# Attention: the turn of the keys put ahead of the first weighted sums, its second part one step on, high queries and back-turning a step up

## The reference, cut to what matters

```python
q_pool = q.reshape(B, H, S // 2, 2, D).mean(axis=3)        # B=4, H=8, S=1152, D=64
scores = scale * np.matmul(q_pool, k.transpose(0, 1, 3, 2))
scores = scores - np.max(scores, axis=-1, keepdims=True)
attn = np.exp(scores)
attn = attn / (np.sum(attn, axis=-1, keepdims=True) + 1e-09)
return np.matmul(attn, v)                                   # 32 heads, 576 x 1152 scores each
...
x = attn_out as rows of 512 numbers                         # 2304 rows
x = moe(x)                                                  # 8 experts, with a skip gate
return moe2(x)                                              # 8 experts, with an output gate
```

## Time and profile before

| what | value |
|---|---|
| median of 3 runs | 1257.56 us |
| profiled execution, its own time | 1266.61 us |
| its span, first to last instruction | 1264.8 us |
| mean granted TensorE clock | 0.952 of full speed |
| head after head, where nothing disturbs | 19.1 us |
| busy in the span: PE, DVE, ACT, POOL | 89%, 60%, 43%, 34% |

### The profile page before, as it was taken

How to read it: one execution, slowest core, us unless ns; L and a number is a source line. 1 busy time by engine, 2 the same in 40 slices (tenths; PEclk the granted TensorE clock), 3 DMA queues, 4 the chain that set the end, 5 groups by cost and what they waited for, 6 DMA issues and landing times.

```text
span 1264.8 us, 21764 instructions
## 1 busy us (share of the span) xinstructions
PE 1128.5 (89%) x7630; PEld 923.3 (73%) x7630; DVE 762.5 (60%) x1710; ACT 545.0 (43%) x945; POOL 435.6 (34%) x335
## 2 busy tenths in 40 slices
PE   6899998889898889988994699999949999999996
PEld 4666676666665666756673699999938999999996
DVE  6565666566667566675655377667654555656551
ACT  2455554445554455443543344444414334443420
POOL 0566555476565666546665100000000000000000
PEclk9799998899999999998998799999978999999998
DMA  4162222132222322223115671318485427141100
GB/s 117 47 190 66 66 58 66 38 97 65 66 50 64 86 66 65 58 57 85 29 30 200 231 276 41 134 59 291 169 319 185 139 85 277 50 159 50 33 17 13
DMA packets 74396, 132.57 MB, mean 105 GB/s; under 512 B 11040, under 2 KB 29472, under 8 KB 74320
## 3 DMA queue, kind: packets, MB, share of 16 engines
q10 hardware_dynamic: 26240, 69.22, 15.2%
q1 hardware_dynamic: 43424, 50.58, 14.8%
q0 software_dynamic: 4656, 11.79, 2.7%
HBM read 106.12 MB, written 19.24 MB: 99 GB/s over the span
## 4 chain that ended last, share of the span: by engine, by line
PE 79%; DVE 13%; ACT 3%; issue 3%; DMA 1%; SPq 1%; POOL 0%; POOLq 0%; another core or an unknown queue 0%; DVEq 0%; ACTq 0%
PE PS L706 22%; PE PS L570 9%; PE PS L491 9%; DVE mx L997 6%; PE PS L553 6%; PE PS L540 6%; PE PS L719 6%; PE PS L720 6%; PE PS L723 6%; PE PS L554 5%; DVE KA L980 2%; DVE KA L977 2%; ACT arena_p L816 1%; PE PS L583 1%; PE PS L607 1%
## 5 line engine op out<-in xcount | busy, mean ns | idle before, releaser
L442 POOL TENSOR_TENSOR arena_a<-arena_a,arena_p 128x576 f32<-128x576 f32 x224 | 323.3, 1443 | 163.6 <-ACT arena_p L816 149.7
L997 DVE TENSOR_REDUCE mx<-PS 128x1 f32<-128x384 f32 (+1 forms) x480 | 250.8, 550 | 146.6 <-PE PS L540 142.4
L706 PE MATMUL PS<-moe,W 128*128 128x128 f32 x2432 | 282.9, 278 | 1.5 <-ACT moe L897 1.5
L706 PEld LDWEIGHTS PS<-moe,W 128*128 128x128 f32 x2432 | 280.0, 194 | 4.0 <-ACT moe L897 2.3
L816 ACT ACTIVATE arena_p<-PS 128x576 f32<-128x576 f32 x288 | 187.3, 651 | 220.1 <-PE PS L554 211.3
L553 PE MATMUL PS<-QHT,KA 128*128 128x288 f32 x576 | 194.2, 340 | 0.4 <-ACT QLT L827 0.4
L540 PE MATMUL PS<-KA,QHT 128*128 128x384 f32 (+1 forms) x480 | 179.0, 376 | 11.2 <-DVE mx L997 10.6
L570 PE MATMUL PS<-arena_p,arena_a 128*64 128x288 f32 x1152 | 170.8, 435 | 7.2 <-DVE R L1065 6.1
L554 PE MATMUL PS<-QLT,KB 65*128 65x288 f32 x576 | 174.3, 306 | 0.0
L1173 DVE TENSOR_TENSOR W2L<-W2R,W2H 128x1024 fp32r<-128x1024 f32 x148 | 171.0, 1217 | 0.7 <-ACT W2H L788 0.7
L788 ACT CAST W2H<-W2R 128x1024 fp32r<-128x1024 f32 x148 | 144.0, 1047 | 46.0 <-PE PS L723 41.3
(11 more groups left out here) (171 smaller groups left out, 1145.7 us busy)
## 6 DMA issues: line engine op xcount, KB each, us to landing
W<-in_moe_w ACTq DMA_DIRECT2D x16, 2048.0 KB, 14.3
W2R<-in_moe_w ACTq DMA_DIRECT2D x16, 2048.0 KB
moe<-xs SPq DMA_DIRECT2D x40, 258.0 KB, 4.3
arena_a<-in_k SPq DMA_DIRECT2D x32, 288.0 KB, 2.9
arena_a<-in_v SPq DMA_DIRECT2D x32, 288.0 KB, 2.8
KB<-KA SPq DMA_DIRECT2D x32, 288.0 KB, 3.1
arena_a<-in_q SPq DMA_DIRECT2D x32, 256.0 KB, 3.1
xs<-padrow ACTq DMA_DIRECT2D x8, 258.0 KB, 3.7
```

Of the source, the lines that this page charges most:

```text
L442: nc.gpsimd.tensor_tensor(Acc[u], Acc[u], P[u][:, t, :], ALU.add).then_inc(acc_step, 1)
L706: last = nc.tensor.matmul(PS[:, HB + f // 4, (f % 4) * PN:(f % 4 + 1) * PN], W1[s][:, d, f * PN:(f + 1) * PN], xT[:, d, :], start=(d == 0) ...
L997: vec.reduce_max(mx3[0:n, t, c:c + 1], PS[0:n, MXB + b % 2, 0:KB_], AX.X).then_inc(pr_max, 1)
```

## The change

Seven things move; no instruction is added or taken away, and the numbers that each computes are the same.

- TensorE: `trans_k(h+2, 0)` stands ahead of the first weighted sums in step 0; `trans_k(h+2, 1)` at the end of step 1 (it was behind the second weighted sums in step 2).
- TensorE: `trans_qh(h+2, 0)` at the start of step 3, `trans_qh(h+2, 1)` at its end (both were at step 4).
- TensorE: the third rough block of one step moves from the end of step 5 to step 4, ahead of the third weighted sums.
- TensorE: `back_values` in step 5 (was 6), `back_sums` between the two halves of step 6 (was 7), `back_logits` at the end of step 6 (was 8).
- ScalarE: `k_high` 0 and 1 and `q_high` ahead of the exponential of step 1; `k_high` 2 ahead of that of step 2; `qh_out` 0 ahead of, and `qh_out` 1 behind, that of step 3.
- VectorE: `k_low` 0 and 1 in slot 1 behind `pool_q` (were in 3 and 4), `k_low` 2 in slot 5 (was 7), `q_low` in slot 7 (was 9).

```diff
--- before.py
+++ after.py
@@ -635,47 +635,45 @@
                 now, after, before = has(h), has(h + 1), has(h - 1)
                 blocks = iter(range(NBLK))
                 for t in range(KT):
-                    if t == 4 and has(h + 2):
+                    if t == 3 and has(h + 2):
                         trans_qh(h + 2, 0)
                     if now:
                         scores(h, t, 0)
                     if after and t < 7:
                         prior(h + 1, next(blocks))
+                    if t == 6 and before:
+                        back_sums(h - 1)
                     if now:
                         scores(h, t, 1)
                     if after and t < 7:
                         prior(h + 1, next(blocks))
                     if t == 0:
+                        if has(h + 2):
+                            trans_k(h + 2, 0)
                         if before:
                             if h - 1 in RANKS_IN:
                                 pe.wait_ge(norm, HEAD_NORM * (h - 2) + 3)
                                 ranks_of_batch(RANKS_IN.index(h - 1))
                             weighted(h - 1, 0)
-                        if has(h + 2):
-                            trans_k(h + 2, 0)
-                    if t == 2:
-                        if before:
-                            weighted(h - 1, 1)
-                        if has(h + 2):
-                            trans_k(h + 2, 1)
+                    if t == 1 and has(h + 2):
+                        trans_k(h + 2, 1)
+                    if t == 2 and before:
+                        weighted(h - 1, 1)
+                    if t == 3 and has(h + 2):
+                        trans_qh(h + 2, 1)
                     if t == 4:
-                        if has(h + 2):
-                            trans_qh(h + 2, 1)
+                        if after:
+                            prior(h + 1, next(blocks))
                         if before:
                             weighted(h - 1, 2)
                             sums(h - 1)
-                    if t == 5 and after:
-                        prior(h + 1, next(blocks))
+                    if t == 5 and before:
+                        back_values(h - 1)
                     if t == 6 and before:
-                        back_values(h - 1)
-                    if t == 7:
-                        if before:
-                            back_sums(h - 1)
-                        if after:
-                            trans_ql(h + 1, 0)
-                            trans_ql(h + 1, 1)
-                    if t == 8 and before:
                         back_logits(h - 1)
+                    if t == 7 and after:
+                        trans_ql(h + 1, 0)
+                        trans_ql(h + 1, 1)
 
             pe.wait_ge(ident_set, 1)
             assert NBLK == 15 and KT == 9
@@ -846,23 +844,21 @@
             def body(h):
                 for t in range(KT):
                     if has(h + 2):
+                        if t == 1:
+                            k_high(h + 2, 0)
+                            k_high(h + 2, 1)
+                            q_high(h + 2)
+                        if t == 2:
+                            k_high(h + 2, 2)
                         if t == 3:
-                            k_high(h + 2, 2)
-                        if t == 4:
                             qh_out(h + 2, 0)
                     if has(h - 1) and t == 5:
                         o_out(h - 1)
                         s_out(h - 1)
                     if has(h):
                         exps(h, t)
-                    if has(h + 2):
-                        if t == 1:
-                            k_high(h + 2, 0)
-                            k_high(h + 2, 1)
-                        if t == 2:
-                            q_high(h + 2)
-                        if t == 4:
-                            qh_out(h + 2, 1)
+                    if has(h + 2) and t == 3:
+                        qh_out(h + 2, 1)
                     if t == 7 and has(h + 1):
                         ql_out(h + 1, 0)
                         ql_out(h + 1, 1)
@@ -1103,13 +1099,11 @@
                     if has(h + 2):
                         if b == 1:
                             pool_q(h + 2)
-                        if b == 3:
                             k_low(h + 2, 0)
-                        if b == 4:
                             k_low(h + 2, 1)
+                        if b == 5:
+                            k_low(h + 2, 2)
                         if b == 7:
-                            k_low(h + 2, 2)
-                        if b == 9:
                             q_low(h + 2)
                     if first is not None and 2 <= b < 2 + RT_STEPS[0]:
                         route_step(first, b - 2)
```

## The result

The changed kernel took 1240.22 us (median of 4 runs, 1235.36 to 1241.71) where the kernel before took 1257.79 (1255.83 to 1262.3). The ratio is 0.9849, with a 95% interval of 0.981 to 0.9888. It is faster, by some 18 to 26 us. The forecast was 1216 with a range of 1196 to 1242: the direction is right, the range holds the time close to its edge, and the gain is less than half of the 42 us forecast by the first comparison, and about 0.6 of it by the pair of traces (1264.8 to 1239.9).

What follows compares the result with a forecast made beforehand. The prediction took TensorE (89% busy) to bound the kernel, its idle time lying in the turning. It summed -1.13 us a head times 30 to -34, plus -8 in routing heads: -42 from 1257.6, about 1216, range 1196 to 1242.

Steps and rivals of the forecast that it cites:

- What bounds it, and which waits go: TensorE bounds; its waits at the ninth tile's turn (0.35 us) and high queries' turn (1.08) go, -1.43 a head.
- My sum: Per-head total of the waits: -1.13 us a head, times 30 gives -34 us.
- The 0.15 for maxima: In step 2, some 0.15 us a head of TensorE's waits for row maxima goes too.
- The copy of the low queries, +0.2: After step 7, its exponential goes ahead of the copy, so the next head's first scores start about 0.2 us late.
- The third rough block, 0: Its 0.21 us wait moves to step 4 with the block; costed at 0, bounds 0.1 gained and 0.4 lost.
- GpSimd beside the query sum, +0.25: At a head's start `pool_q` runs beside GpSimd's last addition, delaying the second key subtraction: +0.25 us a head, bounds 0 and 1.2.
- the second rival: `pool_q` pays the full 1.2 us beside GpSimd in every head: 28 us less gain, 1244 us; chance 0.14.
- The routing heads, -8 beyond the usual saving: In three stretches of three heads, some clock falls stay away: 8 of 39 us saved, bounds 0 and 35.
- Back-turning costed by itself: Moving it a step or more earlier costs 0 in waits for its copies (bounds 0 and 0.1); the low queries' copy pays +0.2.
- The slower rival: TensorE stands 1 to 1.5 us at the end of step 1, its clock falls in each head: about 1300 us; chance 0.06.
- That the clock would stay up in the routing heads: Rival: some 30 of the 39 us there go instead of 8, giving about 1193 us; chance 0.15.

Runs made afterwards that it cites:

- e2: Changed kernel with VectorE's query sum (`pool_q`) made one body earlier, for head h + 3 in slot 9: 1210.70 us, ratio 0.9662 to the kernel before.
- e4: e2 with the waits for the low queries' copy split by part: 1215.13 us, ratio 0.9617 to the kernel before; repeated as e4_again, 1217.49 us, 0.9639.
- e1: Changed kernel with GpSimd's last two additions of each head cut to 8 of 576 columns: 1207.34 us, ratio 0.9628 to the kernel before.
- e7: e4 with all GpSimd additions in the heads around the routing cut to 8 of 576 columns: 1199.97 us, ratio 0.9516 to the kernel before.
- e3: Changed kernel with the back-turning alone put back where the kernel before has it: 1256.44 us, ratio 1.0032 to the kernel before.
- b1: Kernel before with the back-turning alone moved up as in the change: 1252.54 us, ratio 0.9919 to the kernel before.

## Why the prediction was right or wrong

- **What bounds it, and which waits go: right.** The wait at the high queries' turn left every quiet head, TensorE's own work stayed, and with the query sum out of the way the head is 17.75. My sum without the GpSimd term was 19.10 - 1.43 + 0.2 - 0.15 = 17.72. The 0.15 for maxima was not tried alone, and the waits behind maxima as a whole did not shrink: 10.2 us before, 19.5 now, 15.2 in e2. So the close sum doesn't show that this term is right.
- **The copy of the low queries, +0.2: right**, 0.21 by e4.
- **The third rough block, 0: right in size.** TensorE waits 0.21 at it as before, now in step 4. It was not tried alone.
- **GpSimd beside the query sum, +0.25: the step that failed**, in size. It costs 0.66 a head (e1 and e2). I saw the mechanism and had 1.2 as its bound, but I let `pool_q` end at 2.7 to 3.0 after the head's start and the second subtraction at 4.1 to 4.4; they ended at 3.07 and 4.51. I then priced only the ninth tile's turn, which is 0.44 late against e2 and not 0.25. What I left out is the rough block behind it: its maxima stand on VectorE behind the delayed subtractions, so TensorE pays a second time, another 0.22. 0.41 x 30 = 12 us. This was the second rival in kind (VectorE beside GpSimd), at less than its full price, and its 0.14 was too little: the trace had a row of 1.67 for such an instruction, and GpSimd's backlog at the head's end was plain. The measured median lies in that rival's band (1234 to 1254), and the range holds it only because it was drawn into that band.
- **The routing heads, -8 beyond the usual saving: too much.** The excess over nine quiet heads went from 38.95 (210.85 less 9 x 19.10) to 35.7 (201.49 less 9 x 18.42), a gain of 3. The additions are again behind much of it: with the query sum out of their way (e2) the excess is 23.9 (183.62 less 9 x 17.75), 15 under before, and e7 takes 20 us out of the stretches, on e4. VectorE's routing steps now stand among tighter slots, and one was held for 1.46 us. But e4_again has an excess of 38.8 with the query sum out of the way, so these heads depend on more than that, and what it is stays open.
- **Back-turning costed by itself: wrong in kind.** I treated it as a part whose gain is nothing and whose price is 0.2. e3 shows that without it the rest loses 0.25 a head against before instead of gaining 0.68: it is what makes the keys' move pay, in a kernel whose query sum is held up (with the query sum ahead it was not tried), and b1 shows that it shortens the routing stretches alone by 13 us. The two halves can't be added.
- **The slower rival did not come:** its condition, a wait of 1 to 1.5 us at the ninth tile, was not met. With 0.28 us there the clock stayed at 1.00 through seven quiet heads. (Its own sum gives 1306, not 1300.) That the clock would stay up in the routing heads did not come either: it is 0.95, 0.93 and 0.93 after 0.86, 0.95 and 0.88.
- **The sum against the traces.** From the first to the last `divide` it went from 610.91 us (68.80 to 679.71) to 589.56 (63.09 to 652.65), by -21.4: 19 quiet spaces x -0.68 = -12.9, nine in the stretches -9.4, and the last three +0.9. The same by my sum would have been 28 x -1.13 - 8 = -39.6. Of the 18 us that are missing, 8.6 are in the quiet heads, 8.8 in the stretches and 0.9 in the last three. The rest of the span gave 3.5: 5.7 before the first `divide`, where the kernel before itself differs by 3 us between its two traces (68.80 and 65.64), less 2.2 lost behind the last.

## What to carry to other kernels

When work moves earlier on one engine, ask of each instruction what it will now run beside (here the query sum beside GpSimd's additions, 1379 ns instead of 480), and follow a delay on an in-order queue to everybody behind it, not only to the one who waits first. Move what is light and has slack (here a sum of queries, a whole body ahead) out of the contended place rather than the heavy work. And test the halves of a change apart: here each alone lengthened the quiet head, and both together shortened it.

## What was not expected of the hardware

The prediction knew that a VectorE instruction with two operands in SBUF is slow beside a GpSimd addition; how regular and how long it is was not expected. The query sum took 1379 ns in the median of 32 instances where 480 is its own length, and a routing step 1455 against 254. Two instances can be followed: L990 in the earlier trace rows ended 0.36 us behind the end of the addition beside it, and L967 at 297.10 0.35 behind the end of the additions at 298.12. So the instruction seems to be held until a running addition of 1.4 us ends. A subtraction with one operand in PSUM (L973 at 287.17 in e2) kept 0.68 beside an addition that ran until 287.64. The "GPSIMD Engine Reference" of the Trainium skill ("8. Key points") speaks of contention in the case of two SBUF inputs; the runs here agree and put a number on it. The addition can be the one that pays, too: in the kernel before, one that started 0.05 behind L990 took 1.69 us instead of 1.41:

```profile
305.13 0.48 DVE L990 TENSOR_TENSOR arena_a<-arena_a 128x320 fp32r<-128x320 f32 x1
305.18 1.69 POOL L442 TENSOR_TENSOR arena_a<-arena_a,arena_p 128x576 f32<-128x576 f32 x1 [1.07 <-ACT arena_p L816]
```
